# Zero rows after the first group, split loads, and v products on four array tiles

## What is computed

```
for t in range(S):
    cur = einsum('bhd,bhe->bhde', u * k[t], v[t])
    y[t] = einsum('bhd,bhde->bhe', r[t], state + cur)
    state = w * state + einsum('bhd,bhe->bhde', k[t], v[t])
```

## Time and profile before

| | value |
|---|---|
| median of 3 runs | 826.67 us |
| the profiled execution | 826.78 us |
| its span | 825.0 us |
| PE busy | 777.6 us, 94% |
| PE weight loads busy | 714.8 us, 87% |
| VectorE, ScalarE, GpSimd busy | 335.7, 215.4, 335.2 us |
| mean granted PE clock | 0.960 of 2.4 GHz |
| data moved by DMA | 66.91 MB |
| DMA issues: zero fills | 32 of 156.4 KB |
| DMA issues: k, r, v | 48, 48 of 96.0 KB, 24 of 192.0 KB |

### The profile page before, as it was taken

One profiled execution on the slowest core, in us unless ns is written; L12 is line 12 of the kernel. 1 busy time (PEld: TensorE's weight loads), 2 busy tenths in 40 slices (PEclk: granted clock), 3 DMA queues, 4 the chain that ended last, 5 costly groups with the idle time before them and its releaser, 6 DMA issues.

```text
span 825.0 us, 17781 instructions
## 1 busy us (share of the span) xinstructions
PE 777.6 (94%) x7216; PEld 714.8 (87%) x7216; DVE 335.7 (41%) x659; ACT 215.4 (26%) x436; POOL 335.2 (41%) x337
## 2 busy tenths in 40 slices
PE   9888889929999999999899999999999999999995
PEld 8777778729999999999889989989988998998994
DVE  8667565442332233223555333433433433433332
ACT  1234332411221121212132232232232223222221
POOL 6477775426679787977991010010010001001001
PEclk9699887959999999999999999999999999999998
DMA  5666665145653555455440010010000000001001
GB/s 145 184 190 173 178 180 177 59 141 114 129 158 106 136 154 151 108 133 149 110 122 9 1 39 0 1 39 1 1 38 0 0 0 38 0 0 39 1 1 39
DMA packets 42611, 66.91 MB, mean 81 GB/s; under 512 B 11413, under 2 KB 31797, under 8 KB 42549
## 3 DMA queue, kind: packets, MB, share of 16 engines
q1 hardware_dynamic: 28944, 50.76, 22.0%
q10 hardware_dynamic: 10533, 5.80, 3.7%
q0 software_dynamic: 3072, 9.45, 3.1%
HBM read 51.42 MB, written 14.59 MB: 80 GB/s over the span
## 4 chain that ended last, share of the span: by engine, by line
PE 92%; DVE 3%; issue 2%; DMA 1%; POOL 0%; ACTq 0%; ACT 0%; DVEq 0%; POOLq 0%
PE bank L1159 24%; PE bank L1138 24%; PE bank L1083 13%; PE bank L1099 12%; PE ps_y L818 4%; PE ps_y L803 2%; PE ps_x L775 2%; PE ps_s L755 2%; PE ps_x L771 2%; PE ps_l L839 1%; PE ps_x L830 1%; PE ps_s L853 1%; PE ps_m L789 1%; PE bank L1066 1%; DMA rows<-x_rows 1%
## 5 line engine op out<-in xcount | busy, mean ns | idle before, releaser
L1027 POOL DMA_INDIRECT out_rows<-rows,ids_i x24 | 23.1, 962 | 358.7 <-ACT rows L1238 353.2
L1303 DVE TENSOR_TENSOR h_lo<-gf,h_hi 128x512 fp32r<-128x512 f32 x96 | 71.7, 747 | 225.7 <-ACT h_hi L1229 225.7
L134 POOL TENSOR_TENSOR w_lo<-stage,w_hi 128x768 fp32r<-128x768 f32 (+1 forms) x70 | 146.1, 2087 | 5.8
L1159 PE MATMUL bank<-w_hi,h_hi 128*128 128x384 f32 x384 | 130.4, 340 | 1.1 <-DVE h_lo L1303 1.1
L1159 PE MATMUL bank<-w_lo,h_hi 128*128 128x384 f32 x384 | 129.3, 337 | 0.0
L1159 PE MATMUL bank<-w_hi,h_lo 128*128 128x384 f32 x384 | 129.1, 336 | 0.0
L1225 ACT ACTIVATE hc<-bank 128x512 f32<-128x512 f32 x96 | 57.4, 598 | 272.0 <-PE bank L1138 272.0
L1138 PE MATMUL bank<-x_hi,w_hi 128*128 128x512 f32 x288 | 113.4, 394 | 2.4 <-DVE x_lo L1285 2.3
L1138 PE MATMUL bank<-x_lo,w_hi 128*128 128x512 f32 x288 | 113.6, 395 | 0.0
L1138 PE MATMUL bank<-x_hi,w_lo 128*128 128x512 f32 x288 | 113.4, 394 | 0.0
L1266 DVE SCALAR_TENSOR_TENSOR h_lo<-bank,h_hi 128x416 fp32r<-128x416 f32 x64 | 37.8, 591 | 142.0 <-ACT h_hi L1205 142.0
(11 more groups left out here) (166 smaller groups left out, 1202.5 us busy)
## 6 DMA issues: line engine op xcount, KB each, us to landing
stage<-in_moe_w SPq DMA_DIRECT2D x24, 512.0 KB, 6.1
stage<-in_moe_w SPq DMA_DIRECT2D x32, 384.0 KB, 3.1
rows<-x_rows ACTq DMA_DIRECT2D x9, 625.6 KB
x_rows<-pad_row SPq DMA_DIRECT2D x32, 156.4 KB
k_u<-in_k SPq DMA_DIRECT2D x48, 96.0 KB, 2.5
r_u<-in_r SPq DMA_DIRECT2D x48, 96.0 KB, 2.9
v_u<-in_v SPq DMA_DIRECT2D x24, 192.0 KB, 3.4
stage<-in_moe_w_in SPq DMA_DIRECT2D x6, 512.0 KB, 4.1
```

The source lines that it names most:

```text
L134: i = eng.tensor_tensor(w_lo[:, buf, off:off + cols], stage[:, h, 0:cols], w_hi[:, buf, off:off + cols].bitcast(F32), ALU.subtract)
L1159: i = pe.matmul(ps_o[t][:, 0:D], x[:, f % NB, t * P:(t + 1) * P], ww[:, 1, o:o + D], start=f == 0 and x is h_hi and ww is w_hi, stop=f == ...
L1303: dve.tensor_tensor(h_lo[:, f % NB, :], gf[:, f % 2, :], h_hi[:, f % NB, :].bitcast(F32), ALU.subtract).then_inc(gl_ok, 1)
```

## The change

1. **Products with v.** `scores` writes head 1's blocks to the other partition half (`halves[j ^ t]`), so that `am` for head t, block j lies in half j ^ t. v arrives three times over: both heads, and the second head again with its two token halves swapped. `within` is one group of 32 matmuls over row half j ^ t and column half j, with the result where it was; it waits for `masked` and for `from_state` (`f_mm`). The `av_mm` wait is gone, and the `tile` of the first two steps of a chunk stands between `from_state` and `within`.
2. **Loads through a step.** k for step g + 6 is issued once `k_rows(g+1)` is done (`ka_mm`), then zero rows and the piece of weights, then r for step g + 5 after `y_mm` and v after `own_ok`.
3. **Zero rows.** `filled` becomes one semaphore for each expert. During attention only expert 0's four fills are issued. The other 28 go out between the weight pieces of expert 1: four after the second piece, four after each of the next four, eight after the last. `load_x(n)` for n = 0, 1, 2 waits for the fills of expert n, and ScalarE waits for the rest before its loop over groups.
4. **Space.** `ruk` has two buffers instead of three, and the comparison tables of the group table lie in the memory of `am`.

```diff
-        filled = sem("filled")
+        filled = [sem(f"filled{e}") for e in range(E)]
-        ZEROS = E * (U // TR)
+        ZEROS = U // TR
+        def zero_rows(eng, e, n):
+            row = e * RR + n * TR
+            eng.dma_start(x_rows[row:row + TR, :], pad_row[0:TR, :]).then_inc(filled[e], 16)
...
-            ruk = sb("ruk", [P, 3, B, P], stack=st1)
+            ruk = sb("ruk", [P, 2, B, P], stack=st1)
...
             LOAD_AT = {4: 2, 5: 3, 8: 4, 9: 5, 12: 6}
+            ZERO_AT = {2: 0, 3: 1, 6: 2, 7: 3}
...
+                sp.wait_ge(ka_mm, 1)
+                load_k(RB)
                 for g in range(UN):
-                    if g + RB < UN:
-                        sp.wait_ge(y_mm, g + 1)
-                        sp.wait_ge(own_ok, g + 1)
-                        load(g + RB)
-                    for n in range(ZEROS * g // UN, ZEROS * (g + 1) // UN):
-                        zero_rows(n)
+                    if g + 1 + RB < UN:
+                        sp.wait_ge(ka_mm, g + 2)
+                        load_k(g + 1 + RB)
+                    if g in ZERO_AT:
+                        zero_rows(sp, 0, ZERO_AT[g])
                     if g in LOAD_AT:
                         n = LOAD_AT[g]
                         issue_piece(sp, n, n % 2, pc[n])
+                    if g + RB < UN:
+                        sp.wait_ge(y_mm, g + 1)
+                        load_r(g + RB)
+                        sp.wait_ge(own_ok, g + 1)
+                        load_v(g + RB)
...
-                    if g >= 3:
-                        dve.wait_ge(ka_mm, g - 2)
+                    if g >= 2:
+                        dve.wait_ge(ka_mm, g - 1)
...
-                                ins = pe.matmul(ps_s[halves[j], t, b * L:(b + 1) * L], k_u[heads[t], i, b, halves[j]],
+                                ins = pe.matmul(ps_s[halves[j ^ t], t, b * L:(b + 1) * L], k_u[heads[t], i, b, halves[j]],
                                                 r_u[heads[t], i, b, halves[j]], start=True, stop=True)
...
-                def within(g, other):
+                def within(g):
                     i = g % RB
-                    if other:
-                        pe.wait_ge(av_mm, g + 1)
-                    else:
-                        pe.wait_ge(masked, g + 1)
+                    pe.wait_ge(masked, g + 1)
+                    pe.wait_ge(f_mm, g + 1)
                     for b in range(B):
                         for j in range(2):
-                            t = 1 - j if other else j
-                            ins = pe.matmul(ps_y[halves[j], t, b * L:(b + 1) * L], am[halves[j], g % 2, t, b, :],
-                                            v_cols(i, j, t, b, L), start=False, stop=True, skip_group_check=True)
-                    ins.then_inc(y_mm if other else av_mm, 1)
+                            for t in range(2):
+                                ins = pe.matmul(ps_y[halves[j], t, b * L:(b + 1) * L], am[halves[j ^ t], g % 2, t, b, :],
+                                                v_cols(i, j ^ t, 2 * t, b, L), start=False, stop=True,
+                                                skip_group_check=True)
+                    ins.then_inc(y_mm, 1)
...
                     from_state(g)
-                    within(g, False)
...
-                    within(g, True)
+                    within(g)
...
-                def weights(n, b):
+                def weights(n, b, zeros=()):
                     e = entry(sp, group_e, n, E - 1)
                     for i, piece in enumerate(expert_pieces(e)):
                         issue_piece(sp, n * NPE + i, (b * NPE + i) % 2, piece)
+                        for z in zeros[max(i - 1, 0) * ZEROS:i * ZEROS if i < NPE - 1 else None]:
+                            zero_rows(sp, *z)
...
-                weights(1, 1)
+                weights(1, 1, [(z, n) for z in range(1, E) for n in range(ZEROS)])
...
+                    if isinstance(n, int):
+                        act.wait_ge(filled[n], 16 * ZEROS)
                     if isinstance(n, int) and n == 0:
-                        act.wait_ge(filled, 16 * ZEROS)
                         act.wait_ge(scattered, SCATTERS * C)
...
                 group(0, 0)
                 group(1, 1)
+                for e in range(3, E):
+                    act.wait_ge(filled[e], 16 * ZEROS)
...
+    thrice = lambda a: np.concatenate([a, np.roll(a[:, :, :, 1:], P // 2, axis=2)], axis=3)
```

More of the change, by code:

```diff
@@ L220, in attention @@
             region_no = sb("region_no", [P, E], I32, stack=st1)
+            am_f = am[:, :, :, :, :].rearrange("p i t b s -> p (i t b s)")
+            cmp, cmp_s, cmp_t, cmp_n = (am_f[:, i * LOOKS * E:(i + 1) * LOOKS * E].rearrange("p (n e) -> p n e", n=LOOKS)
+                                        for i in range(4))
             ps_s = pb("ps_s", (P, 2, 512), stack=st1)
@@ L259, in attention @@
             v_ok = sem("v_ok")
-            av_mm = sem("av_mm")
+            f_mm = sem("f_mm")
             y_mm = sem("y_mm")
@@ L317, in on_sync, with load_k @@
             def on_sync(sp):
-                def load(g):
+                def load_k(g):
                     (c, q), i = divmod(g, HP), g % RB
@@ L338, in on_sync @@
                         sp.wait_ge(zeros_ok, 1)
-                    load(g)
+                    load_k(g)
+                    load_r(g)
+                    load_v(g)
                 sp.wait_ge(zero_ok, 2)
@@ L741, in on_tensor, with v_cols @@
             def on_tensor(pe):
-                def v_cols(i, j, t, b, cols):
-                    return v_u[halves[j], i, (t * B + b) * DH:(t * B + b) * DH + cols]
+                def v_cols(i, j, n, b, cols):
+                    return v_u[halves[j], i, (n * B + b) * DH:(n * B + b) * DH + cols]
                 def scores(g):
@@ L774, in k_rows @@
                         for j in range(2):
-                            ins = pe.matmul(ps_x[halves[j], KA + 2 * b:KA + 2 * b + sel.shape[1]], ruk[0:R2, g % 3, b, halves[j]],
+                            ins = pe.matmul(ps_x[halves[j], KA + 2 * b:KA + 2 * b + sel.shape[1]], ruk[0:R2, g % 2, b, halves[j]],
                                             sel[0:R2, :], start=True, stop=True)
@@ L802, in from_state @@
                             for t in range(2):
-                                pe.matmul(ps_y[halves[j], t, b * L:(b + 1) * L], r_u[heads[t], i, b, halves[j]],
-                                          x_st[heads[t], q, slot(c, j), b * DH:b * DH + L],
-                                          start=b == 0, stop=False, skip_group_check=True)
-                def within(g, other):
+                                ins = pe.matmul(ps_y[halves[j], t, b * L:(b + 1) * L], r_u[heads[t], i, b, halves[j]],
+                                                x_st[heads[t], q, slot(c, j), b * DH:b * DH + L],
+                                                start=b == 0, stop=False, skip_group_check=True)
+                    ins.then_inc(f_mm, 1)
+                def within(g):
                     i = g % RB
-                    if other:
-                        pe.wait_ge(av_mm, g + 1)
-                    else:
-                        pe.wait_ge(masked, g + 1)
+                    pe.wait_ge(masked, g + 1)
+                    pe.wait_ge(f_mm, g + 1)
                     for b in range(B):
                         for j in range(2):
-                            t = 1 - j if other else j
-                            ins = pe.matmul(ps_y[halves[j], t, b * L:(b + 1) * L], am[halves[j], g % 2, t, b, :],
-                                            v_cols(i, j, t, b, L), start=False, stop=True, skip_group_check=True)
-                    ins.then_inc(y_mm if other else av_mm, 1)
+                            for t in range(2):
+                                ins = pe.matmul(ps_y[halves[j], t, b * L:(b + 1) * L], am[halves[j ^ t], g % 2, t, b, :],
+                                                v_cols(i, j ^ t, 2 * t, b, L), start=False, stop=True,
+                                                skip_group_check=True)
+                    ins.then_inc(y_mm, 1)
                 def logits_of_last(b, d):
```

22 lines of the change are left out of this document (10 added, 12 removed).

## The result

The changed kernel takes 831.34 us (median of 20 runs, 827.0 to 845.07) beside 825.37 us for the kernel before on the same chip (20 runs, 815.78 to 833.17); the ratio is 1.009, interval 1.0067 to 1.0113. The forecast was 822, with 807 to 836 as its range. The change was meant to take 4.5 us and by the ratio cost 7.4, so the sign was wrong. The profiled execution took 830.41 us, its span is 828.7.

The account below looks back on a forecast made before the run. Attention was taken as bound by PE's instruction stream, plus pauses, plus low clock that follows pauses. Attention -12, fill wait +5.5 and low clock +2 gave -4.5 us, so 822 us, range 807 to 836.

Parts of the forecast that it names:

- The four tiles don't serialize: Products with v: four tiles held likelier than the rival of shared-bank serializing, which loses the 11.5 us, 833 us, chance 12%.
- `tile` waits for `a_s`: Ten heavy attention steps: about 0.3 us of waiting for the copy comes up, so each wins 0.3, 3 us in all.
- a late r: Steps 5 and 9 of attention: r behind `issue_piece` lands about 1.5 us late; 2 us charged, bounds nought and 9.8.
- the rest after the first group: Later groups: fills of experts 2 to 7 between weight pieces, and ScalarE's waits for fills 3 to 7, cost nought.
- the fill wait: ScalarE at `load_x(1)`: filled at about 189.7, PE resumes 5.5 us later, plus 2 for low clock.
- so take 0.6 us off each of 24 steps: Attention's products with v: 32 matmuls over four tiles, 14.4 us if nothing else holds, 11.5 us after limits.
- the wider v loads are hidden: Attention's v loads, 192 to 288 KB a step: no cost, since v is asked for four steps ahead.
- the 12 of the forecast: End of attention comes 12 us sooner: 11.5 from products, 2.5 from fills, less 2 for moved loads.
- the rival's 13.3: Rival at the first group: fill wait is the new bound, 8.3 us plus 5 of low clock, 834 us, chance 16%.
- Fills out of attention: Moving 28 of 32 fills out of attention takes 2.5 of the 14 us of PE pauses off.
- Pauses vanish with the fills: Rival in attention: another 7 us of pauses and 5 of low clock go, 810 us, chance 20%.
- `ruk` with two buffers: Attention: it waits for `k_rows(g+1)`, which PE ends before VectorE comes there; priced at nought.

Follow-up runs that it names:

- e2: Kernel before with the products with v over four tiles, triple v and tables in `am`; three `ruk` buffers, old loads and fills; ratio 1.0079.
- e11: Repeat of e2, the kernel before with the tiles part alone; ratio 1.0082.
- e18: Repeat of e9, the kernel before with v loaded three times over and tables in `am`; ratio 1.0073.
- e9: Kernel before with v loaded three times over (288 KB a step, third copy not read) and tables in `am`; ratio 1.0118.
- e1: Kernel before with the change's fills alone: 28 of 32 zero fills moved behind the first group's rows; ratio 1.0051.
- e4: Changed kernel with all 32 fills back in attention at their old steps; ratio to the kernel before 1.0067.
- e8: Kernel before with 24 fills (experts 2 to 7) behind the first group's rows, eight of experts 0 and 1 in attention; ratio 1.0001.
- e17: e9 with its v load issued as two, of 192 KB and 96 KB, both waited for; ratio to the kernel before 1.001.
- e14: Kernel before with tables in `am` and one more 96 KB load of v a step that nothing reads or waits for; ratio 0.9996.
- e15: e2 with the fills of e8, eight in attention and 24 behind the first group's rows; ratio to the kernel before 1.0124.
- e12: e2 with `tile` behind the within-chunk products in place of ahead of them; ratio to the kernel before 1.0118.
- e6: e2 with head t outermost in the products' loops, so two tiles work at a time instead of four; ratio to the kernel before 1.0101.

## Why the prediction was wrong

**Right.** The four tiles don't serialize; `tile` waits for `a_s` (1.4 us over 6 waits, 3 were priced); a late r costs 1.4 us once (2 were priced); the rest after the first group changes by 0.8 us (nought was priced). ScalarE gets past the fill wait 17.1 us after the table (181.30 less 164.18); the forecast was 189.7 less 173.01, 16.7. Part of that is luck: 1 MB at 218 GB/s is 4.8 us and not 4, and with the full 4.6 for the fills and 1.5 for the landing its own terms give 192.3, 19.3 us after the table.

**The step that failed: "so take 0.6 us off each of 24 steps", -11.5 us, and beside it "the wider v loads are hidden".** The matmuls did become that much shorter: PE's busy time from 14 us to the table fell from 134.3 to 121.8. But the part that holds these terms, run alone, is 0.8% slower (e2, e11), 7 us where 11.5 were to be won. Two prices were missing:
- The load that carries the third copy costs 0.7 to 1.2%, 6 to 10 us (e18, e9), as much as the whole tiles part loses, and was priced at nought because v is asked for four steps ahead. That cover is real, but it hides the lateness of v, not what the load does to PE's own instruction stream.
- The clock. The runs of the tiles alone have a granted clock 0.024 (e2) and 0.015 (e11) below before's. Over before's own runs on each of the five chips the time falls by 434 to 566 us for a clock higher by 1 (correlation -0.55 to -0.77); at the two chips' own slopes this stands for 10 and 7 us. Attention's clock was 0.75 to 0.83 in six of the eight profiles with four tiles (0.87 in the changed kernel's, 0.94 with idle matmuls), and 0.90 with two tiles at a time. Prediction and rivals rightly had the clock fall behind idle time, but took it that the shorter group would leave the clock as it was.

-11.5 + 8 + 9 is 5.5 for the 7 measured, which is near for terms of this spread; a part is counted twice, since the wide load alone already has 0.005 to 0.006 of the clock, 2 to 3 us. Against e9 on the same chip e11 is 0.4% faster, within 0.6%: on top of the wide load the four tiles neither win nor lose. The wide load's cost is shown; that it is the clock which eats the tiles' gain is argued. With the idle matmuls the clock came back to 0.94, but these kept PE busy for 15.8 us, so the gain from it was not seen by itself.

In the two profiles of before and after the clock of attention was 0.87 both times, and there attention did end 8.8 us sooner, for the 12 of the forecast. It is not shown that the tiles won this: the fills left attention in that pair too, which e1 and e4 put at 8 us and more, and e8 at 2. A single profile is a rough measure besides: the other profile of before has its table at 167.36 us, 5.6 sooner.

**The fill wait was mis-sized: 7.5 priced, 12 measured** (e1 12.5, the profile after 11.7), near the rival's 13.3. The landing came when it was said. What was missed comes behind it: between `load_x(1)` and `move_ids` ScalarE reads two table entries (L1004), which take 2.35 and 0.72 us, for 0.48 and 0.28 before. `move_ids` follows 4.4 us after `load_x(1)` for 2.1 before, and with it the copies `h_hi`. PE so resumes 8.3 us later for the 5.5 forecast. And the clock stood at 0.50 from 184 to 192, behind a stretch in which PE stood still, so the way from there to the second transposes is 3.4 us longer (23.7 for 20.3) where 2 were priced.

**Fills out of attention: -2.5 priced.** The pauses did not shrink in the changed kernel (12.0 before, 13.2 after). In e8, without the wide load, they did (7.8), yet the whole came out even, 1.0001. By e8 the estimate is right, by e1 it is some 5 us too small; this stays open. "Pauses vanish with the fills" (810) did not come about.

**`ruk` with two buffers was priced at nought** since PE ends `k_rows` first. VectorE waited for it 7 times, 5.9 us. That it costs is not shown: e4 has it and stands no worse than e2, and VectorE's waits for the products fell by 15.5 us.

## What to carry to other kernels

A gain in busy time need not be a gain in time while the granted clock moves, so look at the clock of the busy stretch, before and after, in several runs. A load that nobody waits for need not be free: here the wide one cost 0.7 to 1.2%, and the same load cut in two nothing that could be measured. Look for pauses that end at nothing. A wait that is put in one engine's queue is to be followed to the last thing queued behind it, the reads of table entries too.

## What the runs showed of the hardware

- Four 64 x 64 tiles, two row halves writing one bank in different column halves: 32 matmuls in 0.51 us (42.10 to 42.61), as fast as `from_state`.
- PE's pauses end 1.2 to 1.7 us after a 16 KB packet of the instruction queue, in before and in e9 without exception among those of 0.4 us and more (25), in all profiles 183 of 217.
- Loading v in 128 rows of 2304 bytes instead of 1536 cost 6 to 10 us over 24 steps (e18, e9), and the same bytes in rows of 1536 and 768 bytes nothing that could be measured (e17, e14).
- With four tiles at work attention's mean clock was 0.75, 0.82 and 0.83 of full (e4, e15, e12), but 0.87 in the changed kernel; with two at a time it was 0.90 (e6). Each fall of e4 behind 50 us came behind a pause of PE of 1.49 to 2.04 us.
- ScalarE took 2.35 us to read one table entry (181.91 to 184.26 us, the DMA engines 89% busy), and 0.48 us for the same entry before.
